# Linear attention and two expert stages: the bonus product from PSUM on VectorE, and the early tile list spread over two written-out batches

## The reference

```
attention, per token t:  cur   = (u*k_t) outer v_t
                         y_t   = r_t @ (state + cur)
                         state = w_t * state + k_t outer v_t
first experts:  logits = x @ w_gate + modality_bias[modality_id]
                e = argmax(logits);  out = softmax weight of e * (relu(x @ w1[e]) @ w2[e])
second experts: logits = x @ w_gate + log1p(exp(x @ w_noise)) * noise
                the two best of 8, weights by softmax over the two, results added
```

## Time and profile before

| what | value |
| --- | --- |
| median of 3 runs | 1088.46 us (1087.66 to 1091.93) |
| the profiled execution's own time | 1088.8 us |
| its span, first to last instruction | 1087.0 us |
| mean granted TensorE clock | 0.952 of full |
| PE busy | 963.3 us, 89% |
| DVE busy | 540.9 us, 50% |
| ACT busy | 323.9 us, 30% |
| POOL busy | 413.7 us, 38% |
| chain that ended last, by engine | PE 79%, DVE 10%, issue 5%, POOL 2% |
| attention with the hand-over | 0 to about 204 us |
| the slot table is written (`slot_run`, DVE L1120) | at 251.8 us |
| PE begins the step of the fifth tile | about 256 us |
| tiles of the first and of the second expert stage | 25 and 52 |

### The profile page before, as it was taken

One profiled execution on the slowest core, in us unless ns is written; L12 is line 12 of the kernel. 1 busy time (PEld: TensorE's weight loads), 2 busy tenths in 40 slices (PEclk: granted clock), 3 DMA queues, 4 the chain that ended last, 5 costly groups with the idle time before them and its releaser, 6 DMA issues.

```text
span 1087.0 us, 25044 instructions
## 1 busy us (share of the span) xinstructions
PE 963.3 (89%) x6317; PEld 855.8 (79%) x6318; DVE 540.9 (50%) x890; ACT 323.9 (30%) x561; POOL 413.7 (38%) x443
## 2 busy tenths in 40 slices
PE   5999978799999999755179999999999999999994
PEld 4888867689889888655158889888888988888884
DVE  7888888964533233224755363533534435353331
ACT  2333423323322222124332242422424232242220
POOL 8667753512422222200533343432433344243322
PEclk8999989899999999978579999999999999999998
DMA  6566645119111111144045224152522525222222
GB/s 227 179 196 213 210 159 206 44 35 332 43 37 44 44 36 42 39 153 145 1 146 161 36 62 135 29 159 44 147 48 36 159 44 150 38 44 44 34 41 37
DMA packets 52960, 108.09 MB, mean 99 GB/s; under 512 B 8304, under 2 KB 34672, under 8 KB 52912
## 3 DMA queue, kind: packets, MB, share of 16 engines
q1 hardware_dynamic: 34624, 71.07, 19.3%
q0 software_dynamic: 14400, 31.55, 14.4%
q10 hardware_dynamic: 3888, 4.89, 1.2%
HBM read 82.67 MB, written 24.82 MB: 99 GB/s over the span
## 4 chain that ended last, share of the span: by engine, by line
PE 79%; DVE 10%; issue 5%; POOL 2%; DMA 1%; ACT 1%; POOLq 0%; DVEq 0%; ACTq 0%; SPq 0%
PE ps L1600 20%; PE ps L1601 19%; PE ps L1602 19%; PE ps L1621 6%; PE ps L1512 2%; PE ps L1474 2%; PE ps L1478 2%; DVE grow L873 1%; PE ps L1421 1%; DVE row_mix L1298 1%; PE ps L1444 1%; DVE scores L888 1%; PE ps L1504 1%; PE ps L1537 1%; PE ps L1526 1%
## 5 line engine op out<-in xcount | busy, mean ns | idle before, releaser
L1310 DVE SCALAR_TENSOR_TENSOR hid_lo<-ps,hid_hi 128x512 fp32r<-128x512 f32 x154 | 106.3, 691 | 292.8 <-ACT hid_hi L798 285.3
L1600 PE MATMUL ps<-weights,hid_hi 128*128 (+1 forms) x616 | 215.2, 349 | 8.2 <-issue 6.7
L1600 PE MATMUL ps<-weights,x_hi 128*128 (+1 forms) x462 | 197.7, 428 | 17.6 <-DVE x_lo L1305 9.4
L1602 PE MATMUL ps<-weights,hid_lo 128*128 (+1 forms) x616 | 208.2, 338 | 0.0
L1601 PE MATMUL ps<-weights,hid_hi 128*128 (+1 forms) x616 | 207.8, 337 | 0.0
L1601 PE MATMUL ps<-weights,x_hi 128*128 (+1 forms) x462 | 184.2, 399 | 0.0
L1602 PE MATMUL ps<-weights,x_lo 128*128 (+1 forms) x462 | 183.6, 397 | 0.0
L793 ACT ACTIVATE h_tok<-ps 128x512 f32<-128x512 f32 x154 | 92.2, 599 | 289.9 <-PE ps L1602 281.2
L641 POOL DMA_INDIRECT out_dram<-sy,dst_now x52 | 92.5, 1779 | 210.9 <-DVE sy L1321 200.1
L798 ACT ACTIVATE hid_hi<-ps 128x512 fp32r<-128x512 f32 x154 | 92.2, 598 | 256.3 <-PE ps L1621 251.4
L1600 PEld LDWEIGHTS ps<-weights,hid_hi 128*128 128x128 f32 x616 | 116.6, 189 | 13.6 <-issue 10.4
(11 more groups left out here) (283 smaller groups left out, 1243.8 us busy)
## 6 DMA issues: line engine op xcount, KB each, us to landing
stage<-in_moe_w_dram SPq DMA_DIRECT2D x20, 1536.0 KB, 12.7
kv_in<-in_kv_T_dram SPq DMA_DIRECT2D x24, 512.0 KB, 5.4
kv_in<-in_kv_T_dram SPq DMA_DIRECT2D x24, 448.0 KB, 3.4
w_in<-in_w_T_dram SPq DMA_DIRECT2D x24, 258.5 KB, 4.2
out_dram<-zeros SPq DMA_DIRECT2D x25, 192.0 KB
x_rows<-y_tok ACTq DMA_DIRECT2D x24, 192.0 KB, 4.7
stage<-moe_rows SPq DMA_DIRECT2D x6, 768.0 KB, 4.9
sx<-moe_rows,src_now POOLq DMA_INDIRECT x55
```

Source lines behind the costliest of these rows:

```text
L1310: dve.scalar_tensor_tensor(hid_lo[:, part, :], hT_ps[half], 0.0, hid_hi[:, part, :], ALU.max, ALU.subtract).then_inc(s_hlo[l], 1)
L1600: pe.matmul(out_ps, hi, w_hi, start=first, stop=False)
L1602: return pe.matmul(out_ps, lo, w_hi, start=False, stop=final)
```

## The change

It does six things.

1. The bonus product with v is formed on DVE, straight from PSUM (`bonus_values`), ahead of `y_T` in DVE's step. ACT's copy, POOL's product, the tile `bonus` and the semaphore `s_bnc` go. `rk(g+1)` now waits for the bonus product g of PE alone.
2. The list holds five tiles from 12 chunks. Two batches are written out instead of one, so the loop makes two passes (chunks 0 to 11); `late(b, c)` numbers the written-out chunks from 0.
3. The pieces of the list are spread over chunks 12 to 22: best (12), index (13), PE's product and the expert (15), PE's counts and the places (17), the slots (18), `low_hot` in two halves (19, 20), list product and rows (21). The weight loads go to chunk 15, ACT's four copies to 19 to 22, the gathers of two tiles to 22. In the last step DVE makes `gate_parts` and the picks of chunks 12 to 21 ahead of `bonus_values`.
4. POOL's low part of the first half of w2 (`first_w2`) is made in the last chunk's step, in four pieces.
5. Behind the last chunk, only two chunks are left to pick; PE's counts come after the second x product of tile 0; `first_places` comes after `split_x(1, 1)`.
6. At the start, POOL writes its bf16 tables directly instead of converting them, and two selects for them move behind the first products.

```diff
-    ET, EC = 6, 15
+    ET, EC, EB = 5, 12, 2
...
-            with eng.Fori(0, B - 1) as b:
+            with eng.Fori(0, B - EB) as b:
                 for c in range(NC):
                     step(b, c, False)
-            for c in range(NC):
-                step(B - 1, c, c == NC - 1)
+            for g in range((B - EB) * NC, G):
+                step(g // NC, g % NC, g == G - 1)
+
+        def late(b, c):
+
+            return b * NC + c - (B - EB) * NC if isinstance(b, int) else -1
...
-                if isinstance(b, int) and c == 1:
+                if late(b, c) == 3:
...
-            prime(pool, [s_bv])
             pool.memset(zeros[:, :], 0.0).then_inc(s_const, 1)
             pool.memset(ident[:, :], 0.0)
             pool.memset(causal[:, :], 1.0)
             pool.memset(block_ones[:, :], 1.0)
-            pool.memset(top_row[:, :], 1.0)
+            pool.memset(causal_b[:, :], 0.0)
+            pool.memset(top_row_b[:, :], 1.0)
+            pool.memset(ones_b[:, :], 1.0)
...
-            pool.tensor_scalar(causal_b[:, :], causal[:, :], 1.0, None, ALU.subtract)
-            pool.tensor_copy(iota_s_row_b[:, :], iota_s_row[:, :])
-            pool.tensor_copy(iota_row_b[:, :], iota_row[:, :])
-            pool.tensor_copy(top_row_b[:, :], top_row[:, :])
-            pool.tensor_copy(ones_b[:, :], ones[:, :]).then_inc(s_const, 1)
...
             def product_rk(b, c):
 
                 g, i = b * NC + c, c % NIN
-                pool.wait_ge(s_bnc, 1 + g)
+                if not isinstance(g, int) or g > 0:
+                    pool.wait_ge(s_bn, g)
                 pool.tensor_tensor(rk[:, :, :], r_in[i], k_in[i], ALU.mult).then_inc(s_rk, 1)
...
             def chunk_products(b, c, last):
 
-                g, i = b * NC + c, c % NIN
-                if last:
+                if not last:
+                    product_rk(*after(b, c))
+                if has_after(b, c, 2):
+                    decayed_k(*after(*after(b, c)))
+                if late(b, c) == 10:
                     pool.wait_ge(s_earlyrows, 1)
                     for u in range(2):
                         pool.wait_ge(s_xst[u], 16 + 16 * ((EC + 1 - u) // 2))
                     gather_rows(0, 0, 0, early_src, 0)
                     gather_rows(0, 1, 1, early_src, 1)
-                pool.wait_ge(s_vin[i], 16 * fills(b, c))
-                pool.wait_ge(s_bnc, 1 + g + 1)
-                pool.wait_ge(s_yT, 1 + g)
-                pool.tensor_tensor(bonus_v[:, :, :], vT_in[i], bonus[:, :, :], ALU.mult).then_inc(s_bv, 1)
-                if not last:
-                    product_rk(*after(b, c))
-                if has_after(b, c, 2):
-                    decayed_k(*after(*after(b, c)))
+                if last:
+                    first_w2()
+
+            def first_w2():
+
+                pool.wait_ge(s_hi[0], DONE[0][0])
+                for q in range(4):
+                    part = HALF + q * HALF // 4
+                    done = pool.tensor_tensor(weights[:, W2_LO + part:W2_LO + part + HALF // 4],
+                                              w2_raw[:, part:part + HALF // 4],
+                                              weights[:, W2_HI + part:W2_HI + part + HALF // 4], ALU.subtract)
+                done.then_inc(s_lop[0], 1)
...
+            pool.affine_select(out=causal_b[:, :], in_=causal_b[:, :], compare_op=ALU.is_gt, fill=-1.0,
+                               base=0, pattern=[[1, P]], channel_multiplier=-1)
+            pool.affine_select(out=top_row_b[:, :], in_=top_row_b[:, :], compare_op=ALU.is_equal, fill=0.0,
+                               base=0, pattern=[[0, P]], channel_multiplier=1).then_inc(s_const, 1)
             biases()
             batches(pool, chunk_products)
...
-                if l == 0:
-                    split_w2(0)
-                else:
+                if l == 1:
...
-                act.wait_ge(s_bn, g + 1)
-                act.wait_ge(s_bv, 1 + g)
-                act.activation(bonus[:, :, :], bonus_ps, ACT.Copy).then_inc(s_bnc, 1)
-                if last:
-                    split_piece(0, 0, 0)
-                    split_piece(0, 0, 1)
                 if c < NC - 1:
                     carry(b, c + 1)
-                if isinstance(b, int) and c == NC - 2:
-                    split_piece(0, 0, 2)
-                    split_piece(0, 0, 3)
+                if late(b, c) in (7, 8, 9, 10):
+                    split_piece(0, 0, (2, 3, 0, 1)[late(b, c) - 7])
...
-                early = isinstance(b, int)
-                if early and c == 1:
+                n_late = late(b, c)
+                if n_late == 3:
                     dve.wait_ge(s_earlymm, 1)
                     link(dve.tensor_copy(first_idx[:, :], first_ps))
-                if early and c == 2:
+                if n_late == 5:
                     dve.wait_ge(s_earlymm, 2)
                     link(dve.tensor_tensor_scan(early_seen[:, :], mine_ps[:, EC:2 * EC], ones[:, 0:EC], 0.0,
                                                 ALU.add, ALU.mult))
                     link(dve.tensor_tensor(early_place[:, :], mine_ps[:, 0:EC], early_seen[:, :], ALU.add))
+                if last:
+                    gate_parts()
+                    pick_best(EC, G - 2)
+                    pick_index(EC, G - 2)
+                bonus_values(b, c)
                 dve.wait_ge(s_y, 2 + g + 1)
                 dve.wait_ge(s_bv, 1 + g + 1)
                 dve.tensor_tensor(y_T[:, :, :], y_ps, bonus_v[:, :, :], ALU.add).then_inc(s_yT, 1)
@@ -940,29 +941,47 @@
                     decayed_r(*after(*after(b, c)))
                 if not last:
                     mask_scores(*after(b, c))
-                if early and c == 0:
+                if n_late == 0:
+                    dve.wait_ge(s_const, 5)
                     dve.wait_ge(s_bias, 6)
-                    pick_first(0, EC)
+                    pick_best(0, EC)
+                if n_late == 1:
+                    pick_index(0, EC)
                     dve.tensor_scalar(first_i[:, :], index[:, 0:1], float(E), None, ALU.add).then_inc(s_first, 1)
                     dve.tensor_copy(index_b[:, :], index[:, 0:1]).then_inc(s_early, 1)
-                if early and c == 1:
+                if n_late == 3:
                     early_expert()
-                if early and c == 2:
+                if n_late == 5:
                     early_places()
-                if early and c == 3:
-                    dve.tensor_tensor(low_hot[:, 0:EC, :], low[:, 0:EC].unsqueeze(2).to_broadcast([P, EC, P]),
-                                      iota_row_b[:, :].unsqueeze(1).to_broadcast([P, EC, P]), ALU.is_equal)\
-                       .then_inc(s_early, 1)
-                if early and c == NC - 2:
+                if n_late == 6:
+                    early_slots()
+                if n_late in (7, 8):
+                    early_low(n_late - 7)
+                if n_late == 9:
                     dve.wait_ge(s_earlymm, 3)
                     link(dve.tensor_copy(early_code[:, :], early_ps[:, 0:ET]))
                     dve.tensor_tensor(early_code[:, :], early_ps[:, ET:2 * ET], early_code[:, :], ALU.add)\
                        .then_inc(s_earlyread, 1)
                     dve.wait_ge(s_earlyread, 1)
                     early_rows()
+                if n_late == 10:
                     split_piece(0, 0, 2, DONE[0])
                     split_piece(0, 0, 3, DONE[0])
-                    gate_parts()
+
+            def bonus_values(b, c):
+
+                g, i = b * NC + c, c % NIN
+                dve.wait_ge(s_bn, g + 1)
+                dve.wait_ge(s_vin[i], 16 * fills(b, c))
+                dve.wait_ge(s_yT, 1 + g)
+                dve.tensor_tensor(bonus_v[:, :, :], vT_in[i], bonus_ps, ALU.mult).then_inc(s_bv, 1)
+
+            def early_low(q):
+
+                part = slice(q * EC // 2, (q + 1) * EC // 2)
+                done = dve.tensor_tensor(low_hot[:, part, :], low[:, part].unsqueeze(2).to_broadcast([P, EC // 2, P]),
+                                         iota_row_b[:, :].unsqueeze(1).to_broadcast([P, EC // 2, P]), ALU.is_equal)
+                done.then_inc(s_early, 1)
...
+            def early_slots():
+
                 link(dve.tensor_tensor(high[:, 0:EC], early_place[:, :], low[:, 0:EC], ALU.subtract))
...
-            def pick_first(at, end):
+            def pick_best(at, end):
...
+            def pick_index(at, end):
...
-                pick_first(EC, G)
+                pick_best(G - 2, G)
+                pick_index(G - 2, G)
...
-                    first_places()
                     hidden_low(0, 0)
                     split_x(1, 1)
+                    first_places()
+                    hidden_low(0, 1)
                     first_tiles()
-                    hidden_low(0, 1)
                     first_slots()
...
-                pe.wait_ge(s_bnc, 1 + g)
+                pe.wait_ge(s_bv, 1 + g)
                 for h in range(HP):
```

(26 more changed lines are left out.)

30 lines of the change are left out of this document (10 added, 20 removed).

## The result

The changed kernel takes 1095.71 us (median of 6 runs, 1095.09 to 1097.08); the kernel before took 1088.98 in the runs beside it (6 runs). The ratio is 1.0057, with a 95% interval of 1.0039 to 1.0075: slower by 0.6%, where 1074.1 was forecast. The profiled execution's span is 1093.4 us, against 1087.0.

What follows compares the result with a forecast made beforehand. PE bounds regular loop chunks at 7.07 us and DVE would bound the late stretch. Terms -2.4, -3.5, -7.5, +0.5 and -1.5 sum to -14.4 from 1088.8, adjusted to the median: 1074.1 us, range 1067 to 1085.

Steps and rivals of the forecast that it cites:

- the three signs of being wrong: Loop chunks over 7.2 us, the late stretch over 82, or stages behind 260 us changing their length.
- Bonus on DVE, -2.4 for the loop: Two loop passes: scores come earlier, so short chunks last 6.4 us, 1.2 less a pass; bounds 0 and -5.
- The rival of saturation: DVE saturates everywhere because POOL's products collide with it; 7.9 us a chunk, 1101 us in all, chance 0.06.
- The start, -3.5: Before the first chunks: dropped POOL conversions give 1.7, y_T(0) moves 2.6 earlier; bounds -1.7 and -5.
- The late stretch, -7.5: y_T(12) to y_T(22), with the list spread: 77.1 us against 84.6, DVE its bound; bounds 70 to 83.
- The w_in queued behind them: Late stretch: rest(18) waits for w_in queued behind two weight loads; put at 1 us, bounds 0 and 3.
- 0.6 for a PE wait on the early code: Late stretch: PE waits 0.6 us for the list's early code, read behind grow, r_dec and scores.
- The DVE sum itself, 74.1 and 1.4: Late stretch: ten chunks of 6.3 plus 11.1 of list make 74.1 us; 1.4 unused at chunks 14 and 16.
- Last chunk, +0.5: y_T(22) to y_T(23): 10.5 us against 9.98, between 8.1 undisturbed and 11.6; from -1.9 to +1.6.
- Behind it, -1.5: Behind the last chunk: shorter logits step and PE's count wait gone save 2.8, of which 1.5 kept; bounds 0 and -4.
- "The slot table costed at nothing": Behind the last chunk: slot table wanted one tile earlier, some 4 us after it is written; no cost.
- The clock rival: New waits at chunk 18, 21 and the last one slow the clock; 3 x 2.5 us return, 1081.5 us, chance 0.12.

Runs made afterwards that it cites:

- experiment 1: Changed kernel with the two 1.5 MB weight loads moved behind the chunk's own loads, one per step: 1088.08 us, 0.9984 of the kernel before.
- experiment 4: Kernel before with only the bonus product moved to DVE, ACT's copy and POOL's product gone: 1081.55 us, 0.9941 of the kernel before.
- experiment 7: Changed kernel with the bonus back on ACT and POOL, all other parts kept: 1100.20 us, 1.0094 of the kernel before.
- experiment 2: Changed kernel with DVE's two reads of the early list product moved ahead of grow(23): 1089.56 us, 1.0002 of the kernel before.
- experiments 6: Changed kernel with both the weight loads behind the chunk loads and the list product read ahead of grow(23): 1084.30 us, 0.9943 of the kernel before.
- experiment 12: Repeat of the changed kernel with loads, list reading, old tail order, held zero stores and w2's low part on DVE all mended: 1073.25 us, 0.9839.
- experiment 9: Changed kernel with weight loads, list reading, old order behind the last chunk and held zero stores mended together: 1082.30 us, 0.9926 of the kernel before.
- Experiments 3 and 10: 3: changed kernel, w2's low part on POOL behind the third gather, 1099.79 us. 10: experiment 9 plus that part on DVE and gate_parts later, 1074.82 us.
- experiment 11: Kernel before with the bonus product and the low part of w2 on DVE, the list not spread: 1080.66 us, 0.9916 of the kernel before.

## Why the prediction was wrong

The time missed by 21.6 us, outside the range on its slow side. The late stretch makes 10.8 of it, the last chunk 1.3, the step behind it 4.7, the fifth tile's step 2.3, the stages behind 1.5; 0.9 is that the profiled execution, 1095.09, lies 0.6 below the median, where the forecast took the median as 0.3 below it. Two of the three signs of being wrong came: the late stretch over 82, and stages behind 260 us of another length. Point by point:

- **Bonus on DVE, -2.4 for the loop: right in direction, and near in this trace by luck.** It measured -2.2. All twelve traces with the bonus on DVE have the same loop up to y_T(12), and seven of them gain only 0.7, the mean is 1.3. In all twelve PE waits about 0.94 us for y_T(6), where it waited 0.17 before; in the seven a slow chunk follows (y_T(6) to y_T(7) 7.9 us, in experiment 1 at a granted clock of 0.79), in the other five, the changed kernel's among them, none (6.56 us at 1.00). The two short chunks of a pass take 6.64 and 6.96, not 6.4. The price of 0.69 a product held. The DVE chunk was mis-sized: 41.19 busy in 42.30 is 6.9 a chunk, not 6.3, since `rest` is held by 0.8 and `grow` by 0.4 on an undisturbed 5.56. In the loop that cost nothing: regular chunks stayed at 7.07 with PE as their bound. The rival of saturation, which decides from 7.4 a chunk, did not occur; experiment 4 at 0.9941 speaks against it as well.
- **The start, -3.5: right in size (-3.6), not in its split.** Experiment 4, which keeps POOL's conversions, already has 3.3 of it at y_T(1); experiment 7, which drops them and leaves the bonus on POOL, has 0.4. The tables were given 1.7 and are worth 0.3 to 0.4. y_T(0) came at 17.78, forecast near 17.
- **The late stretch, -7.5: the step that failed.** What failed were two small terms set beside the DVE sum. "The w_in queued behind them ... I put 1, bounds 0 and 3": the wait was 3.52 on DVE and 4.08 on PE, and without it the stretch is 7.65 us shorter (8.05 where experiment 2's edit is in too). "0.6 for a PE wait on the early code": 2.77, and without it the stretch is 5.6 shorter (6.0 where experiment 1's edit is in too). Both were priced as DVE's delay alone. Each wait of PE was paid about twice, as the prediction itself had read in the earlier trace rows for the kernel before and then used in a rival only: the window 123.92 to 144.07 ran at a clock of 0.75, the same two chunks of experiment 1 at 1.00. PE waits for the code because in its order of work the gate product stands behind `s_earlyread`, and on DVE grow, r_dec and scores (3.1 us) stood ahead of the reading. The rows to add up were there. The DVE sum itself, 74.1 and 1.4, came out near the 74.26 and 74.07 of experiments 6 and 12 by errors that cancel. In experiment 12 the chunks' operations take 57.1 us, not 63, and the list 14.1, not 11.1; DVE is idle for 4.1, not 1.4. The list was read too small before, too: its operations there take 12.3, not 9.3.
- **ACT's pieces, cost nothing: no run speaks against it.** They lie in ACT's idle time in the traces read, as at 155.53 in that of experiment 9. No run tried them by themselves.
- **Last chunk, +0.5: the size was wrong.** 11.74, at the end named as "with all four quarters in the way 11.6". Experiments 3 and 10 show what holds it there: POOL's run of pieces held a DVE operation for its full length. The value taken, between 8.1 and 11.6, assumed that cutting gives DVE turns. PE's wait of 6.70 in that chunk was not priced at all; the slow clock behind it falls into the next stretch.
- **Behind it, -1.5: wrong in sign, +3.2.** The prediction named what is late next ("the DVE list up to high_is") and the idle time in front of it, and then gave it no price. The new order puts `first_places` behind two steps that wait for PE and ACT: 3.9 us of idle DVE. With the old order the gain over before is 1.4 (28.2 against 29.57), which is the forecast figure. So the reordering costs 4.6, and without it the forecast figure is met. That fewer picks alone earn it is not shown, since the slow clock behind the longer wait for y_T(23) stands in the same stretch.
- **"The slot table costed at nothing": the table was in time, and the step of the fifth tile still grew by 2.3.** ACT's register reads ran beside the zero stores, since a list of five tiles makes them begin one tile earlier. The forecast looked for a wait on a semaphore and not for a slower reading.
- **The clock rival (0.12)** had the mechanism that decided: "if the new waits at chunk 18, 21 and the last one each set one off". It put 2.5 on each and left out the waits themselves, and it took them off a gain of 14, not off the size of the waits.
- **Behind the thirteenth `hid_hi`** the stages are 1.5 longer. The second gate iteration stood at a clock of 0.85 there and 1.00 before (15.30 against 14.10 us). The same stretch scatters from 792.6 to 795.6 over the kernels, none of which touches it. Its cause wasn't tried.

The difference between PSUM and SBUF sources in the Trainium skill's table ("VectorE: DVE Perf Modes", the TRN2 errata) is not borne out in the changed kernel either: 0.69 for `bonus_v` with a PSUM source, 0.69 for `r_dec` without one.

The change thus contains a good kernel: experiment 12 is 1.6% faster than before. Against experiment 11 on the same chip it gains 7.4 us, which is what spreading the list over two batches, with the tables and the moved picks, is worth once its large waits are gone and the stores held back. With the waits in, the same spreading costs about 13 (ratio 1.0057 against experiment 4's 0.9941).

## What to carry to other kernels

When pieces of a side task are moved into a tight loop, walk each queue that they pass and name the first instruction behind them: here a chunk's load behind 3 MB of weights, a gate product behind a reading, a list behind another engine's step. Together they cost more than the spreading is worth without them. Where TensorE is near its bound, price its waits at about twice their length if the trace of before shows the clock falling behind such a wait; the two of 4.08 and 2.77 cost that here, and the one of 0.94 in the loop nothing or 1.5 us, from trace to trace. And measure a change of six parts by part: the bonus product alone gave 0.6%, and the others gained only after five places in them were mended.

## What the runs showed of the hardware

A run of GpSimd products one behind the other held a VectorE operation with two SBUF inputs for the whole run: 4.60 us for a step of 0.24 beside four pieces of 3.83 in all, and 7.39 for two splits of 3.42 beside 3.85. In both cases the VectorE operation had begun first, by 0.66 and 0.24 us, and still ended behind the last piece. The Trainium skill ("SBUF — State Buffer", the section on the two separate sides) says that the pair of ports which VectorE and GpSimd share is locked for one whole instruction, by whichever starts first, and the other engine blocks. The blocking agrees; that the first to start has the pair does not, and here it lasted over four instructions, with no turn between them.

While 25 stores of zeros were being issued (19.04 us), reads of one table entry into a register on ACT took 0.81 to 1.21 us; with the stores held back they took 0.28 to 0.49, and 0.45 to 0.70 for the reads that then fell beside the stores.

A load of a chunk's w issued behind 3 MB of weights on the same queue landed 12.5 us after its issue, where 3.8 is this load's median on the page; the weights were first used four chunks on.
